# Attention scores by head on the two row halves of the array, and a row sum's small term three columns wide

## What is computed

```python
scores = scale * np.matmul(q, k.transpose(0, 1, 3, 2))
rel = pos[:, None] - pos[None, :]
mask = (rel >= 0) & (rel < 128)
scores = np.where(mask, scores + bias[None], -1000000000.0)
scores = scores - np.max(scores, axis=-1, keepdims=True)
attn = np.exp(scores)
attn = attn / (np.sum(attn, axis=-1, keepdims=True) + 1e-09)
attn_out = np.matmul(attn, v)
# then, on x = attn_out as (2304, 512):
x = sigmoid(x @ w_gate) * (x @ w_val) @ w_out
x = ((x @ w1) * (x @ w2) @ w3) @ w2_out
```

## Time and profile before

| | |
|---|---|
| median of 3 runs | 971.4 us (971.06 to 971.5) |
| profiled execution, its own time | 972.31 us |
| its span in the profile | 970.5 us |
| TensorE, busy | 899.5 us (93%) |
| GpSimd, busy | 722.3 us (74%) |
| VectorE, busy | 689.1 us (71%) |
| ScalarE, busy | 505.8 us (52%) |
| granted clock of TensorE, mean | 0.979 |

### The profile page before, as it was taken

How to read it: one execution, slowest core, us unless ns; L and a number is a source line. 1 busy time by engine, 2 the same in 40 slices (tenths; PEclk the granted TensorE clock), 3 DMA queues, 4 the chain that set the end, 5 groups by cost and what they waited for, 6 DMA issues and landing times.

```text
span 970.5 us, 15723 instructions
## 1 busy us (share of the span) xinstructions
PE 899.5 (93%) x5272; PEld 869.0 (90%) x5272; DVE 689.1 (71%) x1506; ACT 505.8 (52%) x1139; POOL 722.3 (74%) x535
## 2 busy tenths in 40 slices
PE   3999989868999997999999999799999999989998
PEld 3889877767899997899889999789988999988998
DVE  7988899885666668577756666857785666686666
ACT  4888878767544443544454444354444444435441
POOL 6778877876887775998679777489867977738940
PEclk9999999979999999999999999999999999998999
DMA  7333432410222210222142222012113211211301
GB/s 235 105 108 113 121 95 78 143 47 23 86 76 78 66 66 22 72 82 69 41 140 79 66 83 71 22 66 87 66 44 131 87 66 66 67 42 52 102 1 66
DMA packets 37409, 75.92 MB, mean 78 GB/s; under 512 B 3153, under 2 KB 16081, under 8 KB 37329
## 3 DMA queue, kind: packets, MB, share of 16 engines
q1 hardware_dynamic: 37328, 74.92, 23.9%
HBM read 68.09 MB, written 6.82 MB: 77 GB/s over the span
## 4 chain that ended last, share of the span: by engine, by line
PE 71%; DVE 14%; ACT 7%; issue 5%; POOL 2%; DMA 1%; SPq 0%; ACTq 0%; DVEq 0%; POOLq 0%
PE quad_ps L424 15%; PE quad_ps L426 14%; PE quad_ps L425 14%; PE o_ps L424 8%; PE o_ps L426 8%; PE o_ps L425 8%; DVE rowsum L766 3%; DVE xs_lo L811 2%; ACT exps L584 2%; DVE negs L755 1%; DVE xf L879 1%; POOL prob L1007 1%; ACT pt_hi L595 1%; DVE pt_lo L775 1%; ACT wq_hi L630 1%
## 5 line engine op out<-in xcount | busy, mean ns | idle before, releaser
L424 PE MATMUL quad_ps<-xs_hi,wq_hi 128*128 128x384 f32 x840 | 286.9, 342 | 25.4 <-ACT s L646 22.0
L426 PE MATMUL quad_ps<-xs_hi,wq_lo 128*128 128x384 f32 x840 | 284.6, 339 | 0.0
L425 PE MATMUL quad_ps<-xs_lo,wq_hi 128*128 128x384 f32 x840 | 284.5, 339 | 0.0
L424 PEld LDWEIGHTS quad_ps<-xs_hi,wq_hi 128*128 128x128 f32 x840 | 160.8, 191 | 31.7 <-issue 16.5
L1041 POOL TENSOR_TENSOR wq_lo<-wsum,wq_hi 128x1280 fp32r<-128x1280 f32 x60 | 177.3, 2955 | 9.4 <-ACT wq_hi L630 9.4
L424 PE MATMUL o_ps<-h_hi,wo_hi 128*128 128x384 f32 x480 | 161.2, 336 | 3.2 <-DVE xf L879 3.1
L425 PEld LDWEIGHTS quad_ps<-xs_lo,wq_hi 128*128 128x128 f32 x840 | 160.7, 191 | 0.0
L426 PEld LDWEIGHTS quad_ps<-xs_hi,wq_lo 128*128 128x128 f32 x840 | 160.5, 191 | 0.0
L426 PE MATMUL o_ps<-h_hi,wo_lo 128*128 128x384 f32 x480 | 160.4, 334 | 0.0
L425 PE MATMUL o_ps<-h_lo,wo_hi 128*128 128x384 f32 x480 | 160.4, 334 | 0.0
L1037 POOL TENSOR_TENSOR wq_lo<-raw_q,wq_hi 128x512 fp32r<-128x512 f32 x60 | 77.7, 1295 | 105.8 <-ACT wq_hi L624 105.8
(11 more groups left out here) (89 smaller groups left out, 1893.8 us busy)
## 6 DMA issues: line engine op xcount, KB each, us to landing
raw_q<-w SPq DMA_DIRECT2D x24, 512.0 KB, 3.5
raw_q<-w_gate SPq DMA_DIRECT2D x18, 512.0 KB, 3.5
raw_q<-w_val SPq DMA_DIRECT2D x18, 512.0 KB, 3.5
raw_o<-w_out SPq DMA_DIRECT2D x18, 512.0 KB, 3.5
raw_o<-w_times_wout SPq DMA_DIRECT2D x12, 512.0 KB, 3.6
k_raw<-kT SPq DMA_DIRECT2D x16, 288.0 KB, 2.9
q_raw<-qT SPq DMA_DIRECT2D x16, 288.0 KB, 3.0
v_raw<-v SPq DMA_DIRECT2D x16, 256.0 KB, 2.7
```

Source lines behind the costliest of these rows:

```text
L424: pe.matmul(out, lh, rh, start=start, stop=False, skip_group_check=onto)
L425: pe.matmul(out, lh, rl, start=False, stop=False, skip_group_check=onto)
L426: return pe.matmul(out, ll, rh, start=False, stop=stop, skip_group_check=onto)
```

## The change

- A step is no longer two blocks of 64 queries for both heads but 128 queries for each **head** `h`. The stationary operand is the head's 64 partitions of `q_hi` or `q_lo` by 128 queries, the moving one the same 64 partitions of `k_hi` or `k_lo` by up to 256 keys. The six products of a step alternate between the heads, and so between the lower and the upper 64 rows of the array. Head 0 writes bank `pA[0]`, head 1 `pA[1]`, in every step.
- So `scores(n)` waits until step n-1 has been read by DVE, where it waited for step n-2.
- `KW` is 256: DVE, ACT and POOL work on 256 keys for each head. The first step of a pair has 128 keys for each head, the last has 64 rows by 192 keys for each head.
- `q_hi` and `q_lo` are plain 128x576 operands. `q_hi` is one copy on ACT in a pair's second slot, `q_lo` one subtraction on POOL in that slot; DVE's half is gone, and so are the large memsets (four of 128x64 remain).
- The bias table is stored for every head, 128x8x256 instead of 128x4x192.
- The row sums have three columns for a buffer, two sums and one constant 1.0, and the small term is added to all three; the reciprocal takes two of them.

```diff
-QB = 64
-NQ = S // QB
-KW = WINDOW + QB
+KW = WINDOW + P
+SP = (S + P - 1) // P * P
...
             def scores(n):
-                buf, pb = n % 2, pair % 2
+                pb = pair % 2
...
-                wait(pe, scored, n - 1)
-                first = max(0, i - 1) * P
-                last = min(S, first + 2 * P)
-                for j in blocks_of(i):
-                    q = slice((2 * i + j) * P, (2 * i + j + 1) * P)
-                    mm = product(pA[buf][:, j * 2 * P:j * 2 * P + last - first],
-                                 (q_hi[pb][:, q], q_lo[pb][:, q]),
-                                 (k_hi[pb][:, first:last], k_lo[pb][:, first:last]))
+                wait(pe, scored, n)
+                keys, q = keys_of(i), slice(i * P, (i + 1) * P)
+                first, last = (i - 1) * P + keys.start, (i - 1) * P + keys.stop
+                sides = ((q_hi, k_hi), (q_hi, k_lo), (q_lo, k_hi))
+                for k, (left, right) in enumerate(sides):
+                    for h in range(2):
+                        rows = slice(h * D, (h + 1) * D)
+                        mm = pe.matmul(pA[h][:, keys], left[pb][rows, q], right[pb][rows, first:last],
+                                       start=k == 0, stop=k == 2)
...
-                if i in (1, 2):
+                if i == 1:
                     act.wait_ge(q_in, 16 * (pair + 1))
-                    h = i - 1
-                    nc.scalar.copy(diagonal(q_hi[pb], h), blocks(q_raw, h)).then_inc(q_hi_done, 1)
+                    wait(act, qk_done, STEPS * (pair - 1))
+                    nc.scalar.copy(q_hi[pb][:, 0:S], q_raw[:, :]).then_inc(q_hi_done, 1)
...
-                if i == 2:
-                    dve.wait_ge(q_hi_done, 2 * pair + 2)
-                    nc.vector.tensor_tensor(out=diagonal(q_lo[pb], 1), in0=blocks(q_raw, 1),
-                                            in1=diagonal(q_hi[pb], 1), op=ALU.subtract).then_inc(q_split[1], 1)
...
-                nc.vector.tensor_scalar(rowsum2[:, cols], rowsum[:, cols], 1e-9, None, ALU.add).then_inc(sum_done, 1)
+                nc.vector.tensor_scalar(rowsum2[0:rows, 3 * buf:3 * buf + 3], rowsum[0:rows, 3 * buf:3 * buf + 3],
+                                        1e-9, None, ALU.add).then_inc(sum_done, 1)
...
-            nc.vector.memset(q_hi[0][:, :].bitcast(F32), 0.0)
-            nc.vector.memset(q_lo[0][:, :].bitcast(F32), 0.0).then_inc(zeroed[0], 1)
+            nc.vector.memset(rowsum[:, :], 1.0)
+            for b in range(2):
+                nc.vector.memset(q_hi[b][:, S:SP].bitcast(F32), 0.0)
+                op = nc.vector.memset(q_lo[b][:, S:SP].bitcast(F32), 0.0)
+            op.then_inc(zeroed[0], 1)
```

More of the change, by code:

```diff
@@ L116, in build @@
             v_raw = sb(one, "v_raw", [P, VC * P], F32)
-            q_hi = [sb(one, f"q_hi{b}", [P, NQ * P], F32R) for b in range(2)]
-            q_lo = [sb(one, f"q_lo{b}", [P, NQ * P], F32R) for b in range(2)]
+            q_hi = [sb(one, f"q_hi{b}", [P, SP], F32R) for b in range(2)]
+            q_lo = [sb(one, f"q_lo{b}", [P, SP], F32R) for b in range(2)]
             k_hi = [sb(one, f"k_hi{b}", [P, S], F32R) for b in range(2)]
@@ L122, in build @@
             v_lo = [sb(one, f"v_lo{b}", [P, VC * P], F32R) for b in range(2)]
-            bias = sb(one, "bias", [P, HP * KW], F32)
+            bias = sb(one, "bias", [P, H * KW], F32)
             eye = sb(one, "eye", [P, P], F32)
@@ L126, in build @@
             exps = [sb(one, f"exps{b}", [P, 2 * KW], F32) for b in range(2)]
-            prob = [sb(one, f"prob{b}", [P, 2 * (2 * P + QB)], F32) for b in range(2)]
+            prob = [sb(one, f"prob{b}", [P, 2 * KW], F32) for b in range(2)]
             pt_hi = [sb(one, f"pt_hi{b}", [P, 4 * P], F32R) for b in range(2)]
@@ L315, in load_q @@
             def load_q(p):
-                for split in q_split:
-                    wait(sp, split, p)
+                wait(sp, q_split, p)
                 sp.dma_start(q_raw[:, :], qT[p]).then_inc(q_in, 16)
@@ L581, in exponentials @@
                 wait(act, norm_done, n - 1)
[L582 to L586, removed]
+                rows = rows_of(i)
+                for h in range(2):
+                    op = nc.scalar.activation(heads(exps[buf])[0:rows, h, keys_of(i)],
+                                              heads(negs[buf])[0:rows, h, keys_of(i)], ACT.Exp, scale=-1.0,
+                                              bias=negmax[0:rows, 2 * buf + h:2 * buf + h + 1],
+                                              accum_out=rowsum[0:rows, 3 * buf + h:3 * buf + h + 1])
                 op.then_inc(exp_done, 1)
@@ L751, in score @@
                 buf = n % 2
[L752 to L754 removed]
+                rows, keys = rows_of(i), keys_of(i)
+                for h in range(2):
                     op = nc.vector.tensor_tensor_reduce(
[L756 to L758 removed]
+                        heads(negs[buf])[0:rows, h, keys], pA[h][0:rows, keys],
+                        heads(bias_of(pair))[0:rows, h, keys], -SCALE, 3.0e38, ALU.add, ALU.min,
+                        negmax[0:rows, 2 * buf + h:2 * buf + h + 1])
                 op.then_inc(scored, 1)
@@ L997, in normalise @@
                 wait(pool, turned, n - 1)
[L998 to L1010, removed]
+                rows, keys = rows_of(i), keys_of(i)
+                op = nc.gpsimd.tensor_tensor(
+                    out=heads(prob[buf])[0:rows, :, keys], in0=heads(exps[buf])[0:rows, :, keys],
+                    in1=recip[0:rows, 2 * buf:2 * buf + 2].unsqueeze(2).to_broadcast([rows, 2, keys.stop - keys.start]),
+                    op=ALU.mult)
                 op.then_inc(norm_done, 1)
```

64 lines of the change are left out of this document (29 added, 35 removed).

## The result

The changed kernel takes **1019.9 us** (median of 4 runs, 1016.1 to 1021.2) against 971.3 of the kernel before: 4.9% slower, ratio 1.0494 with a 95% interval of 1.0466 to 1.0522. The forecast was 963.4, and the range of 955 to 990 does not hold it. In what follows each kernel is given by its median and by its ratio to the kernel before in the same job (970.9 to 972.4 us).

A forecast was written before the change was run, and what follows sets the result against it. No engine clearly bound the 80 steps; VectorE's 1e-9 addition led the chain of waits. Chain: -24.5 - 7.3 + 11 + 1.9 + 0.5 = -18.4; loop: -11 to -4; taken: -8, so 971.4 - 8 = 963.4 us, range 955 to 990.

The forecast's parts named there:

- The new wait: Scores(n) on TensorE waiting until VectorE has read step n-1: 0.5 us, only in the first steps.
- the sum of the loop: ScalarE's round with VectorE over a pair's five slots: 11.9 us a pair, 203 to 210 for 216 us, with start -11 to -4.
- Rival C: ScalarE's loop and the tighter wait take all that VectorE's waits gave: 970 to 973 us, chance 0.12.
- The three columns: VectorE's 1e-9 addition on three columns costs 0.15 us like one column, without waiting for GpSimd: 24.5 us off the chain.
- Rival A: Three columns of VectorE's 1e-9 addition wait for GpSimd as two do: +15, 986 us (977 to 996), chance 0.37.
- the chain's -24.5 us: Time leaving the chain of waits if VectorE's 1e-9 addition no longer waits for GpSimd.
- The widths: Wider exponentials (ScalarE), scores (VectorE) and normalisation (GpSimd), with last steps' second tiles: 4.7 + 4 + 2.4, 11 us onto the chain.
- The transposes: TensorE's transposes keep their sizes; 16 in a pair, counted as 1.6 us.
- The start: The larger bias table, 384 to 1024 KB, delays the loads behind it by 1.9 us.
- TensorE's products: With both row halves at work at once, TensorE takes 10.3 us for a pair, one after another 11.6, against 12.7.
- Rival B: Row halves don't work at once and changes between 64 and 128 rows drain TensorE's array: +10, 981 us, chance 0.10.

The follow-up runs named there:

- the kernel with four banks: The changed kernel with a head's score steps alternating between two banks, scores waiting for step n-2, fold and pv one bank each: 992.5 us, ratio 1.0216.

## Why the prediction was wrong

*The parts, one by one, in the kernel before:* the tighter wait +34.4, the widths and the table +12.7 (the table 3.1 of it), the third column +4.9, in sum +52.0 against the +48.6 of the whole change. What is left, -3.4, holds the parts' effects on each other, the small gains (q_lo off VectorE, one cast fewer on ScalarE, the products at the two row halves behind a wait) and, on the other side, the second tile of a pair's last step; these were not tried apart.

**The new wait** is the step that failed. The prediction gave it 0.5 us, for the first steps, and said that "in the steady part the wait ends while TensorE would be a little ahead". It cost 34.4 us. The text before it named the right things (pv, transposes and fold behind the wait, ScalarE behind the transposes, VectorE behind ScalarE), but priced only the wait and not the way that those make. In the sum of the loop ScalarE's queue was taken as full in two slots of five and as waiting for VectorE alone in the others, with pv and transposes always done in time. The round at 106.6 to 111 shows them on the path: 0.62 for the scores, 0.94 for pv, then pv's copy and the cast of the transposes, and ScalarE's wait for pv rose from 2.9 to 41.6 us with the tighter wait alone. Rival C had this mechanism ("the loop through ScalarE and the tighter wait") at far too low a price and ended at no change.

**The three columns** are the second step that failed: they were taken as free with a little over even chances, against the rule that was quoted there. The rule held: 721 and 562 ns. Rival A, which gave +15 us in all for it, had the place and the sign; its own price for the third column, 6 + 3 us, was 4.9 in the kernel before. Its 986 us fell short since the wait above is not in it. Of the chain's -24.5 us a form without the wait gives what else binds lets through: 14 us in the kernel before, where TensorE is nearly full, and 30 in the changed one.

**The widths** were right in the size of each tile: 0.05 us more on ScalarE and 0.07 on VectorE for 0.06, 0.19 on GpSimd for 0.21. Their price was too low. The run of the widths has no second tile in a pair's last step; without the terms for it the prediction's shares of the chain give about 6 us (6.9 / 3 + 6.5 / 3 + 10 / 6), and 12.7 less the table's 3.1 are 9.6. That the 12.7 lie so near to the prediction's 11 + 1.9 is luck: the 11 hold the second tiles, which were not measured. The transposes did not keep their number either: two more for each pair (288 in all for 256), and the sum counts 16 transposes as 1.6 us where four at 0.35 make 1.4.

**The start**, 1.9 us, measured 3.1 by total time, whose interval of 1.1 to 3.7 holds it. In the changed kernel line 755 first begins at 19.02 us, 2.6 later than before, for the 2.4 of table and first wait.

**TensorE's products**: both halves work at once, as taken, but with the queue full the two changes of mode eat all of it (1.10 us for 1.07), so TensorE's 10.3 us for a pair had about 1.3 us too little (an estimate: the prediction's 2.9 for its 1.6). Rival B's price for a change was 0.16 us; about 0.2 is seen. Its point, that TensorE's queue passes 12.7 us for a pair, never came to decide, since TensorE idles.

## What to carry to other kernels

When a buffer is no longer doubled, price the instructions queued behind the new wait and not the wait: follow them once round through every engine back to the same wait. If a wait must stay, put work that doesn't need it ahead of it in the queue; here that was worth 30 us, about what the wait had cost, without another buffer. And when a small instruction on VectorE takes many times the 0.15 us of its one-column form and ends with a GpSimd instruction, as line 755 did, look for a form without the wait (here one column at a time), or leave it out, before adding work around it.

## What the runs showed of the hardware

- The small addition waits for GpSimd with two columns and with three (726 and 721 ns on the mean), and not with one (146). The Trainium skill (Vector Engine (DVE) Microarchitecture Reference, "5.1 Performance modes — why throughput varies by op and dtype") counts an odd outermost size as fit for the two-port mode if source and result match; the three columns bear that out. One wait can outlast several GpSimd instructions: the line's instruction at 119.68 took 2.38 us and ended at 122.06, with the third of three that lay back to back on GpSimd (ends 119.81, 120.81, 122.04). With 64 rows the mean was 1212 ns; whether the rows or the place in the pair make that was not tried apart (the same 16 steps, with 128 rows, averaged 771 in the kernel before with three columns).
- Products on the two row halves of the array start in pairs, even where the program puts three of one half ahead of three of the other (110.24, 110.46 and 110.58, two each). The Trainium skill (TensorE: Matmul & The Clock Gate, "What overlaps and what doesn't" in Part 3) has products begin in strict program order; the run with the order by heads does not agree.
- A change between 64 and 128 rows, with TensorE's queue full, costs about 0.1 us ahead of it and 0.1 behind it. In the kernel with four banks the fold's last product holds the first scores by 0.33 us for 0.23 in the kernel before, and these hold the next by 0.22 for 0.12; from the scores to pv it is 0.21 and 0.22 for 0.12 each. For a group of six products with 256 columns, by halves, that took the whole gain.
- The first product behind a wait of TensorE holds the next by 0.22 us in place of 0.12 with 128 rows throughout, too (18 groups of the kernel with the tighter wait alone, between 16 and 125 us).
